# Weights of a dense mixture of experts prepared with more lead

## What is computed

```python
# 1. attention with hashed buckets, 16 heads (2 x 8) of 768 tokens, 64 wide
mask = q_bucket[:, :, :, None] == k_bucket[:, :, None, :]      # 6 bits from q @ proj > 0
attn = softmax(where(mask, q @ k.T / 8, -1e9));  x = attn @ v   # -> x: 1536 tokens x 512
# 2. dense mixture: every expert for every token, gates P by Sinkhorn (8 rounds)
for e in range(8):                                             # w1: 512 x 1024, w2: 1024 x 512
    out += P[:, e:e+1] * (maximum(x @ w1[e], 0) @ w2[e])
# 3. routed mixture: each token goes to the expert of its largest logit, if x @ w_skip > 0
y[mask_e] = gate * (maximum(xc[mask_e] @ w1[e], 0) @ w2[e])
```

## Time and profile before

| | |
|---|---|
| median of 3 runs | 1511.65 us (1511.47 to 1511.9) |
| profiled execution | 1508.9 us, span 1507.0 us |
| granted TensorE clock, mean | 0.951 of 2.4 GHz |
| PE busy | 1334.1 us (89%), 12075 matmuls |
| DVE, ACT, POOL busy | 947.9, 764.1, 686.5 us (63, 51, 46%) |
| DMA | 154.8 MB, 103 GB/s over the span |

### The profile page before, as it was taken

The page is one execution under the profiler, slowest core; times in us unless marked ns, Lnnn a source line. Parts: engine busy times, 40 slices in busy tenths (PEclk is TensorE's granted clock), DMA queues, the critical chain, the costliest instruction groups (busy, mean ns, idle before and its releaser), DMA issues.

```text
span 1507.0 us, 31277 instructions
## 1 busy us (share of the span) xinstructions
PE 1334.1 (89%) x12075; PEld 1029.8 (68%) x12075; DVE 947.9 (63%) x1540; ACT 764.1 (51%) x1429; POOL 686.5 (46%) x859
## 2 busy tenths in 40 slices
PE   7888889987999889889988989888899998998998
PEld 4555556765448767777866778776778887556765
DVE  6777779753746656566655656565565564557984
ACT  6777779844224444344444434444444456323762
POOL 4555656732335754555665555664554440021211
PEclk9888889999999999999999999999999999999999
DMA  8333332015342134214122412322240012257860
GB/s 191 96 87 90 95 88 55 30 62 178 92 157 92 48 88 141 77 53 130 50 78 77 155 53 78 87 93 78 77 141 1 15 57 85 84 207 275 306 239 19
DMA packets 128692, 154.83 MB, mean 103 GB/s; under 512 B 9248, under 2 KB 88648, under 8 KB 128560
## 3 DMA queue, kind: packets, MB, share of 16 engines
q1 hardware_dynamic: 126096, 149.63, 32.9%
q0 software_dynamic: 2240, 3.35, 0.6%
q10 hardware_dynamic: 224, 0.02, 0.0%
HBM read 115.59 MB, written 39.36 MB: 103 GB/s over the span
## 4 chain that ended last, share of the span: by engine, by line
PE 38%; POOL 19%; DVE 14%; ACT 12%; DMA 7%; issue 6%; SPq 3%; ACTq 0%; POOLq 0%; DVEq 0%
PE ps L1949 4%; DMA w_parts<-w2a 4%; PE ps L2024 3%; PE ps L2048 3%; PE ps L2028 3%; PE ps L2027 3%; PE ps L2050 3%; PE ps L2049 3%; POOL parts L858 3%; ACT w_out L1062 3%; DVE h_ring L1539 2%; POOL parts L856 2%; ACT parts L1092 2%; PE ps L1937 2%; POOL parts L853 2%
## 5 line engine op out<-in xcount | busy, mean ns | idle before, releaser
L2048 PE MATMUL ps<-x,w 128*128 128x256 f16 x1344 | 376.5, 280 | 87.1 <-ACT parts L1106 59.7
L2049 PE MATMUL ps<-x,w 128*128 128x256 f16 x1344 | 376.2, 280 | 0.0
L2050 PE MATMUL ps<-x,w 128*128 128x256 f16 x1344 | 375.7, 280 | 0.2 <-issue 0.2
L2107 PE MATMUL ps<-w_seven,h_ring 128*128 128x256 f16 x1008 | 277.2, 275 | 21.2 <-ACT ps L1182 14.2
L2109 PE MATMUL ps<-w_seven,h_ring 128*128 128x256 f16 x1008 | 277.0, 275 | 0.0
L2108 PE MATMUL ps<-w_seven,h_ring 128*128 128x256 f16 x1008 | 276.9, 275 | 0.0
L2048 PEld LDWEIGHTS ps<-x,w 128*128 128x128 f16 x1344 | 134.3, 100 | 133.5 <-ACT parts L1106 68.8
L2050 PEld LDWEIGHTS ps<-x,w 128*128 128x128 f16 x1344 | 135.0, 100 | 18.9
L2049 PEld LDWEIGHTS ps<-x,w 128*128 128x128 f16 x1344 | 134.5, 100 | 16.6
L853 POOL TENSOR_TENSOR parts<-parts 128x256 f32<-128x256 f32 x72 | 62.6, 870 | 178.4 <-ACT parts L1101 178.4
L2107 PEld LDWEIGHTS ps<-w_seven,h_ring 128*128 128x128 f16 x1008 | 99.3, 99 | 39.7 <-ACT ps L1182 15.9
(11 more groups left out here) (265 smaller groups left out, 3287.1 us busy)
## 6 DMA issues: line engine op xcount, KB each, us to landing
w_ready<-w_out SPq DMA_DIRECT2D x48, 448.0 KB, 4.3
w_seven<-w_ready SPq DMA_DIRECT2D x42, 512.0 KB, 4.4
w_parts<-w1a SPq DMA_DIRECT2D x128, 128.0 KB, 2.7
w_parts<-w2a SPq DMA_DIRECT2D x48, 256.0 KB, 4.5
w_in<-w1b SPq DMA_DIRECT2D x4, 2048.0 KB, 8.8
w_in<-w2b SPq DMA_DIRECT2D x4, 2048.0 KB, 9.6
w_in_b<-w1b SPq DMA_DIRECT2D x4, 2048.0 KB, 10.9
w_in_b<-w2b SPq DMA_DIRECT2D x4, 2048.0 KB, 9.7
```

The costliest lines, as they stand in the source:

```text
L2048: pe.matmul(acc, w_hi, x_hi, start=(opens and kt == 0), stop=False, skip_group_check=not opens)
L2049: pe.matmul(acc, w_hi, x_lo, start=False, stop=False, skip_group_check=not opens)
L2050: last = pe.matmul(acc, w_lo, x_hi, start=False, stop=(kt == 1), skip_group_check=not opens)
L2107: pe.matmul(acc[:, p, :], a_hi, b_hi, start=begins, stop=False, skip_group_check=True)
```

## The change

1. *Attention.* In `load_pair` the loads of w1 units go behind both moves of marks, one unit in each of rounds 2 to 7, and `first_units` on GpSimd follows that.
2. *Blank rows.* Four DMAs of 7, 7, 7 and 5 row tiles, in SP's list of experts 2 to 5 behind the store of piece 1, in place of one.
3. *Expert 1's weights*, prepared during expert 0's second product: per step the w2 piece before the w1 quarter, on VectorE at every third tile.
4. *Experts 2 to 6.* The next w2 piece is loaded ahead of the store of the one before. Piece 0 of the next expert is loaded in batch 1 and summed in batch 2 of the expert before, piece 2 summed in batch 0. On ScalarE and VectorE the first w2 piece of a batch comes at the start of the seven-product and the w1 quarter of batch 1 later in it. Fills are spread otherwise between the w1 loads.
5. *Expert 0's groups.* `first_expert_step` on VectorE runs inside `group`, before its two additions, and no longer behind them.

```diff
@@ -89,6 +89,7 @@
...
 RING = 4
+BLANK_PARTS = tuple(slice(first, first + 7) for first in range(0, SLOTS // P - 7, 7)) + (slice(21, SLOTS // P),)
 PARTS = 4
@@ -517,28 +518,25 @@
...
-            def load_pair(j, behind_even=()):
+            def load_pair(j, units=()):
                 load_stack(2 * j, 0)
...
                 load_v(2 * j, 0)
-                for unit in behind_even:
-                    load_w1(0, unit // 2, unit % 2)
                 move_marks(2 * j - 1, 1)
...
                 move_marks(2 * j, 0)
+                for unit in units:
+                    load_w1(0, unit // 2, unit % 2)
             for j in range(1, G // 2):
-                load_pair(j, {1: (0, 1), 2: (2,), 3: (3,), 4: (4,), 5: (5, 6), 6: (7,)}.get(j, ()))
+                load_pair(j, {1: (0, 1)}.get(j, (j,)))
             move_marks(G - 1, 1)
...
             load_plain_w2(0, 1)
-            sp.wait_ge(blank_ready, 3)
-            sp.dma_start(row_tiles, blank[:, :].unsqueeze(1).to_broadcast([P, SLOTS // P, ROW])
-                         ).then_inc(blanked, 16)
             load_plain_w2(0, 2)
@@ -548,43 +546,54 @@
...
                 if n + 1 < FQ:
+                    load_w2(1, n + 1)
+                store_w2(1, n)
+                if n + 1 < FQ:
                     load_w1(1, n + 1, 0)
                     load_w1(1, n + 1, 1)
-                store_w2(1, n)
-                if n + 1 < FQ:
-                    load_w2(1, n + 1)
             for k in (1, 7, 6, 2, 4, 5, 3):
                 fill_w2(1, k)
+            load_w2(2, 0)
+            def blank_rows(part):
+                sp.wait_ge(blank_ready, 3)
+                tiles = BLANK_PARTS[part]
+                sp.dma_start(row_tiles[:, tiles, :],
+                             blank[:, :].unsqueeze(1).to_broadcast([P, tiles.stop - tiles.start, ROW])
+                             ).then_inc(blanked, 16)
...
                 seven = e < E - 1
-                if seven:
-                    load_w2(e, 0)
                 load_w1(e, 0, 0)
...
                 if seven:
+                    load_w2(e, 1)
                     store_w2(e, 0)
-                    load_w2(e, 1)
+                    load_w2(e, 2)
                     store_w2(e, 1)
-                    load_w2(e, 2)
+                if e - 2 < len(BLANK_PARTS):
+                    blank_rows(e - 2)
+                if seven:
+                    load_w2(e, 3)
+                    store_w2(e, 2)
                 load_w1(e, 1, 0)
...
                 if seven:
-                    store_w2(e, 2)
-                    load_w2(e, 3)
+                    if e + 1 < E - 1:
+                        load_w2(e + 1, 0)
                     store_w2(e, 3)
-                    for k in (1, 7, 6):
-                        fill_w2(e, k)
+                    fill_w2(e, 1)
                 load_w1(e, 2, 0)
...
                 if seven:
-                    for k in (2, 4, 5):
+                    for k in (7, 6):
                         fill_w2(e, k)
...
                 if seven:
-                    fill_w2(e, 3)
+                    for k in (2, 4, 5, 3):
+                        fill_w2(e, k)
@@ -765,7 +774,7 @@
...
-            first_units = {(1, 1): 0, (2, 1): 1, (3, 1): 2, (4, 0): 3, (4, 1): 4, (5, 1): 5, (6, 1): 6, (7, 1): 7}
+            first_units = {(1, 1): 0, (2, 1): 1, (3, 1): 2, (4, 1): 3, (5, 1): 4, (6, 0): 5, (6, 1): 6, (7, 1): 7}
@@ -858,34 +867,39 @@
...
             for n in range(FQ):
+                sum_w2(1, n)
                 for kt in range(2):
                     sum_w1(1, n, kt)
-                sum_w2(1, n)
+            def sum_quarter(e, i):
+                for kt in range(2):
+                    sum_w1(e, i, kt)
...
                 sum_h(g)
-                if g % FQ != 0 or g == FIRST_SEVEN:
+                n, place = divmod(g - FQ, FQ)
+                if n < NB - 1 or (n == NB - 1 and place == 0):
                     continue
-                ahead, batch = (g - FQ) // GE + 1, (g - FQ) // FQ % NB
-                if batch == 0:
-                    if ahead < E - 1:
-                        sum_w2(ahead, 0)
+                ahead, batch = n // NB + 1, n % NB
+                seven = ahead < E - 1
+                if place == 0 and batch == 0:
+                    if seven:
                         sum_w2(ahead, 1)
-                    for kt in range(2):
-                        sum_w1(ahead, 0, kt)
-                elif batch == 1:
-                    if ahead < E - 1:
-                        sum_w2(ahead, 2)
+                    sum_quarter(ahead, 0)
+                elif place == 0 and batch == 1:
+                    if seven:
                         sum_w2(ahead, 3)
-                    for kt in range(2):
-                        sum_w1(ahead, 1, kt)
-                else:
-                    for i in (2, 3):
-                        for kt in range(2):
-                            sum_w1(ahead, i, kt)
-            for i in (2, 3):
-                for kt in range(2):
-                    sum_w1(E - 1, i, kt)
+                    sum_quarter(ahead, 1)
+                elif place == 0:
+                    sum_quarter(ahead, 2)
+                    sum_quarter(ahead, 3)
+                elif place == 1 and batch == 0 and seven:
+                    sum_w2(ahead, 2)
+                elif place == 1 and batch == 2 and ahead + 1 < E - 1:
+                    sum_w2(ahead + 1, 0)
+            sum_quarter(E - 1, 2)
+            sum_quarter(E - 1, 3)
@@ -1164,19 +1183,17 @@
...
                 finish(left)
-                if batch > 0:
-                    for kt in range(2):
-                        w1_part(ahead, batch - 1, kt)
+                if batch == 2:
+                    quarter(ahead, 1)
+                elif ahead < E - 1:
+                    w2_part(ahead, 2 * batch)
                 act.wait_ge(seven_done, seven_count(n, 7))
...
                 act.activation(s_out[:, :, 0, :], s_pairs[2], ACT.Copy).then_inc(su2_kept, 1)
-                if batch == 2:
-                    for kt in range(2):
-                        w1_part(ahead, 2, kt)
-                elif ahead < E - 1:
-                    w2_part(ahead, 2 * batch)
+                if batch > 0:
+                    quarter(ahead, 2 * batch - 2)
                 act.wait_ge(seven_done, seven_count(n, 5))
@@ -1190,9 +1207,8 @@
...
                 for n in range(FQ):
-                    for kt in range(2):
-                        w1_part(1, n, kt)
                     w2_part(1, n)
+                    quarter(1, n)
@@ -1544,10 +1560,11 @@
...
-            def group(g, todo):
+            def group(g, todo, extra=lambda: None):
...
                     h_low(earlier)
+                extra()
                 dve.wait_ge(products_done, product_count(g, 4))
@@ -1562,26 +1579,34 @@
...
+            def quarter(e, i):
+                for kt in range(2):
+                    w1_part(e, i, kt)
             def seven(n, todo):
...
                 ahead, batch = e + 1, n % NB
-                for g in todo:
+                for g in todo[:-1]:
                     h_low(g)
-                if batch > 0:
-                    for kt in range(2):
-                        w1_part(ahead, batch - 1, kt)
+                if batch == 2:
+                    quarter(ahead, 1)
+                elif ahead < E - 1:
+                    w2_part(ahead, 2 * batch)
+                h_low(todo[-1])
                 dve.wait_ge(seven_done, seven_count(n, 2))
...
                     add_gated(e, tiles + 2 * p, slice(0, XH), s_pairs[0][:, p, :], s11_added)
-                if batch < 2 and ahead < E - 1:
-                    w2_part(ahead, 2 * batch)
+                if batch == 1:
+                    quarter(ahead, 0)
+                elif batch == 2:
+                    w1_part(ahead, 2, 0)
                 dve.wait_ge(seven_done, seven_count(n, 4))
...
                 if batch == 2:
-                    for kt in range(2):
-                        w1_part(ahead, 2, kt)
+                    w1_part(ahead, 2, 1)
@@ -1649,13 +1674,10 @@
...
                                               ALU.mult).then_inc(regated, 1)
-                    if first and 1 <= t <= 2 * FQ:
-                        n = (t - 1) // 2
-                        if t % 2 == 1:
-                            for kt in range(2):
-                                w1_part(1, n, kt)
-                        else:
-                            w2_part(1, n)
+                    if first and t % 3 == 1:
+                        w2_part(1, t // 3)
+                    elif first and t % 3 == 2:
+                        quarter(1, t // 3)
                     if last:
@@ -1790,12 +1812,10 @@
...
                     ready = [g for g in todo if g < k - 1]
-                    group(k, ready)
+                    group(k, ready, lambda: first_expert_step(k) if k < GE else None)
                     todo = [g for g in todo if g >= k - 1] + [k]
...
```

(2 more changed lines are left out.)

5 lines of the change are left out of this document (4 added, 1 removed).

## The result

Over four runs of each kernel the changed one takes 1379.0 us (1375.2 to 1380.7) against 1511.8 (1511.5 to 1516.8): a ratio of 0.911, 95% interval 0.908 to 0.914. The forecast was 1356 us, in a range of 1338 to 1390. The profiled execution took 1377.9 us, its span is 1376.0, 131.0 us shorter than before. The question is thus where 25 us of the forecast 156 stayed.

The account below looks back on a forecast made before the run. TensorE, busy 1334 of 1507 us, was taken as the bound, so only its waits and half clock could be won. 105 - 10 - 2.5 + 44.7 + 9.2 + 5 + 4.5 = 155.9 us gained gave 1356 us, range 1338 to 1390.

Parts of the forecast that it names:

- 105 us for the batches' old waits: Experts 1 to 5: 15 batches each lose 7.0 us to waits for prepared weights and half clock; all 105 us gained.
- 10 us for the added sum: w2 sum between two sums of h on GpSimd delays the next sums; 1.1 us lost nine times, 10 us.
- the 16 that I got by this rule: Added w2 sums on GpSimd: if every one took the long form beside VectorE, 16 us lost instead of 10.
- 2.5 us for expert 2's first piece: GpSimd's sum for this piece waits for its load behind 7 w2 fills: 2.5 us lost once (0 to 5).
- 44.7 us in attention: Masks no longer queue behind w1 loads on SyncE; five pairs of heads take 28.56 us, not 37.50: 44.7 us gained.
- 9.2 and 5 us in expert 0: Blank rows no longer delay raw w2 piece 2: 9.2 us gained; VectorE's step ahead of its additions: 5 us gained.
- 4.5 us in the second product: Expert 0's second product: TensorE's column-sum wait on VectorE and half clock behind it go; 4.5 us gained (2.8 to 5).
- two of the signs: Experts 1 to 5: batches of 38 to 39 us, clock near 1.00; waits of some 1 us for product 7's copy.
- The second piece: Rival, experts' batches: landing and sum take 5 us more, ScalarE blocks TensorE in 10 batches; +43, 1399 us; chance 0.13.
- GpSimd as the bound: Rival, groups: added sum's delay passes through three groups and costs its full 4.3 us nine times; +29, 1385 us; chance 0.15.
- The masks: Rival, attention: w1 work on GpSimd, not SyncE, holds the next head; half the gain gone, +22, 1378 us; chance 0.05.
- the lead: Rival, batches: preparing pieces a batch ahead fails, early parts block ScalarE and VectorE; slower than before, 1554 us; chance 0.02.

Follow-up runs that it names:

- the sum at place 3: Changed kernel with the added w2 sum on GpSimd behind the fourth group's sum of h instead of the second's, all work done: 1349.7 us, ratio 0.891.

## Why the prediction was right, and where it was not

The time was 23 us above the forecast and inside the range. By the steps of the sum, with what the runs show:

- *105 us for the batches' old waits:* 97. With the added sum taken out of the way the 15 batches take 572.6 to 572.8 us, not 564.8. A batch 2 takes 38.4 us and more (39.6 in expert 1), the others 37.8 to 38.1; I had given all of them expert 6's 37.65. Of the 8 us left 5.2 stand in the five batches 2, where TensorE waits by 0.15 to 0.8 us in several spots; what would remove them was not tried.
- *10 us for the added sum:* 25, shown by leaving it out and by moving it. **This is the step that failed, in size.** The mechanism, its place and its nine batches were as I wrote, and so, nearly, was the room: I had 2.30 + 0.2 = 2.5 us, and the whole sum leaves 2.8. What was wrong is the length: I let the sum take 2.9 us, or 4.3 at worst; it takes 5.05 in all nine. The 4.3 was one sum of the kernel before (476.01 to 480.34), in which two operations were long, 1.17 and 1.70 us, of which I named only the second. I also left out the clock, some 7.4 us in the nine together, and that the sum of h behind can be held up too (3.56 us for 2.84).
- The Trainium skill (GPSIMD Engine Reference, Specifications) has GpSimd contend with VectorE instructions of two SBUF inputs. I chose 10 us against the 16 that I got by this rule; the traces side with the rule, and go beyond it.
- *2.5 us for expert 2's first piece:* TensorE waits 2.95 us at 405.65, for the same reason as in the nine batches; with the sum at place 3 that wait is gone.
- *44.7 us in attention:* 45.8, and 45.2 by itself. Nothing was late next.
- *9.2 and 5 us in expert 0:* 7.7 and 4.1, together 11.75 where I had 14.2; undone by themselves, 6.6 and 4.1. The four parts of the blank rows, for which I had under 5 us each, take a median of 10.4 us to land (8.0 the last); nothing waited for them. The waits of the step that I priced at 0 are most of the 6.8 us for VectorE's addition (2.09 of them belong to an x split); a group later they vanish.
- *4.5 us in the second product:* its stage gained 2.5 net of the 2.95 above, so 5.4.
- *The end:* counted as 0, it took 1.0 longer.

Together: 97.2 - 25.2 - 2.95 + 45.8 + 11.75 + 5.45 - 1.0 = 131.05 us, against 155.9.

The range held, but two of the signs that I had named for being right did not come: the 15 batches take 39.86 us each and not 38 to 39, at a clock of 0.98, and the waits for the copy of product 7 are 2.2 us and more, not some 1 us.

The rivals. The second piece isn't late in the changed kernel: waits for the copy of product 6 are 2.6 us in all. But it was nearer than I held, since 2.6 us later is enough for 18 us of loss, and I had called the order of store and load a saving of 1.27 us. GpSimd as the bound came nearest in time (1385) and not in kind: the delay ends within one group, as GpSimd's idle 1.52 us before the next sum of h (527.65) shows, and the same work elsewhere costs nothing. The masks did not stay late, and the lead does form: ScalarE no longer waits for the high part of a piece in a batch of experts 1 to 5.
